# Input weights of a gated mixing network brought in by output halves, the products begun one unit sooner, and the low-rank factors loaded later

## What is computed

```python
scores = (q @ k.T) / 8 + bias            # 8 heads of 64, local window of 96 keys and 8 global keys
x = softmax(where(keep, scores, -1e9)) @ v          # then heads side by side: x is (2, 768, 512)
h = relu(x @ w_in)                                  # (512, 1024)
u, v = h[..., :512], h[..., 512:]
v_n = (v - mean(v)) / sqrt(var(v) + 1e-6)           # per token
x = (u * (w_spatial @ v_n + b_spatial)) @ w_out
u = x + V.T @ (U.T @ x)                             # along the tokens, rank 32
out = u + relu(u @ w_ch1) @ w_ch2                   # 512 -> 2048 -> 512
```

## Time and profile of the kernel before

| | |
|---|---|
| runs | 557.4, 559.49, 560.1 us |
| the profiled execution | 562.82 us, of which the span of instructions is 560.7 us |
| mean granted TensorE clock | 0.980 of full speed |
| busy, of the span | TensorE 95%, VectorE 52%, ScalarE 31%, GpSimd 20% |
| DMA | 36.25 MB, mean 65 GB/s; the q1 queue (SyncE's) 39776 packets |
| TensorE's waits listed after 118 us | 4.7 us in five groups: for VectorE's x_lo 1.6, uT_lo 1.0, gv_lo 0.9, gated 0.8, and issue 0.4 |
| first 130 us | TensorE busy 112.9 us, VectorE 95.9 us, ScalarE 75.3 us, GpSimd 41.0 us |

### The profile page before, as it was taken

How to read it: one execution, slowest core, us unless ns; L and a number is a source line. 1 busy time by engine, 2 the same in 40 slices (tenths; PEclk the granted TensorE clock), 3 DMA queues, 4 the chain that set the end, 5 groups by cost and what they waited for, 6 DMA issues and landing times.

```text
span 560.7 us, 7652 instructions
## 1 busy us (share of the span) xinstructions
PE 533.7 (95%) x2728; PEld 418.3 (75%) x2728; DVE 289.5 (52%) x845; ACT 174.3 (31%) x429; POOL 112.0 (20%) x134
## 2 busy tenths in 40 slices
PE   7688999899999999999989999999999999999996
PEld 5455666567777788878768888888888888888884
DVE  5748888857775534689822265523146524011012
ACT  4755665645555533332311101021010102101010
POOL 5884000000000001498389500000000000000000
PEclk8969999989999999999989999999999999999999
DMA  7975454545514000055223100002000002000002
GB/s 179 226 158 130 102 102 105 119 97 130 122 47 129 29 30 0 2 168 161 84 76 112 39 0 1 0 1 75 1 0 2 0 2 75 1 0 1 0 1 79
DMA packets 45835, 36.25 MB, mean 65 GB/s; under 512 B 29504, under 2 KB 39744, under 8 KB 45792
## 3 DMA queue, kind: packets, MB, share of 16 engines
q1 hardware_dynamic: 39776, 19.34, 15.6%
q0 software_dynamic: 3216, 11.63, 6.9%
q10 hardware_dynamic: 2800, 4.72, 2.9%
HBM read 32.54 MB, written 3.15 MB: 64 GB/s over the span
## 4 chain that ended last, share of the span: by engine, by line
PE 80%; DVE 10%; POOL 4%; issue 3%; DMA 2%; ACT 1%; DVEq 0%; POOLq 0%; ACTq 0%
PE ps L1255 66%; PE ps L1228 5%; PE ps L1299 4%; PE ps L1272 4%; DVE uT_first L1051 2%; DMA w_raw<-in_moe_w_in 2%; POOL win_lo L464 2%; DVE pr L923 1%; PE ps L1390 1%; POOL win_hi L462 1%; DVE uT_lo L1058 1%; DVE wspT_lo L1010 1%; DVE sc L907 1%; DVE gv_lo L991 1%; POOL small L486 0%
## 5 line engine op out<-in xcount | busy, mean ns | idle before, releaser
L1176 DVE SCALAR_TENSOR_TENSOR hT_lo<-ps,hT_hi 128x512 fp32r<-128x512 f32 x48 | 33.2, 692 | 171.4 <-ACT hT_hi L773 171.4
L773 ACT ACTIVATE hT_hi<-ps 128x512 fp32r<-128x512 f32 x48 | 28.8, 599 | 228.2 <-PE ps L1255 228.2
L597 ACT ACTIVATE pr<-sc,small 128x256 f32<-128x256 f32 (+1 forms) x96 | 46.2, 483 | 52.2 <-DVE small L907 46.8
L907 DVE CUSTOM_DVE_ANT_0 sc<-ps,bias 128x256 f32<-128x256 f32 (+1 forms) x96 | 35.0, 400 | 22.8 <-PE ps L1272 21.2
L1255 PE MATMUL ps<-win_hi,xT_hi 128*128 128x512 f32 x96 | 40.9, 427 | 0.0
L1051 DVE STREAM_TRANSPOSE ys<-tokens 32x128 f32<-32x128 f32 x128 | 38.7, 302 | 1.8
L1255 PE MATMUL ps<-uT_hi,w1a_hi 128*128 128x512 f32 x96 | 38.0, 396 | 1.0 <-DVE uT_lo L1058 1.0
L1255 PE MATMUL ps<-win_hi,xT_lo 128*128 128x512 f32 x96 | 38.5, 401 | 0.0
L1255 PE MATMUL ps<-win_lo,xT_hi 128*128 128x512 f32 x96 | 38.4, 400 | 0.0
L1255 PE MATMUL ps<-uT_lo,w1a_hi 128*128 128x512 f32 x96 | 38.1, 397 | 0.0
L1255 PE MATMUL ps<-uT_hi,w1a_lo 128*128 128x512 f32 x96 | 38.0, 396 | 0.0
(11 more groups left out here) (154 smaller groups left out, 1096.4 us busy)
## 6 DMA issues: line engine op xcount, KB each, us to landing
w_raw<-in_moe_w_ch POOLq DMA_DIRECT2D x16, 512.0 KB, 4.0
wsp<-in_moe_w_spatial ACTq DMA_DIRECT2D x12, 384.0 KB, 3.7
vn<-in_v SPq DMA_DIRECT2D x12, 256.0 KB, 3.7
out<-ys SPq DMA_DIRECT2D x12, 256.0 KB, 2.2
qk_late<-in_q SPq DMA_DIRECT2D x24, 112.0 KB, 3.5
qk_late<-in_k SPq DMA_DIRECT2D x24, 112.0 KB, 3.7
vp<-in_v SPq DMA_DIRECT2D x10, 224.0 KB, 4.5
w_raw<-in_moe_w_in POOLq DMA_DIRECT2D x4, 512.0 KB, 6.0
```

Source lines behind the costliest of these rows:

```text
L597: act.activation(pr[:, k % 3, e, 0:w], sc[:, k % 2, e, 0:w], ACT.Exp, bias=nmax[:, k % 2, e:e + 1], scale=-1.0, accum_out=sums[:, k % 3, e ...
L773: act.activation(hT[0][:, n % 2, :], h1_ps(n), ACT.Relu).then_inc(s["hT_hi"], 1)
L907: dve.tensor_tensor_reduce(out=sc[:, k % 2, e, 0:w], in0=scores_ps(k, e)[:, 0:w], in1=bias[:, 2 * p + e, WINDOW - w:WINDOW], scale=-SCALE, ...
L1176: dve.scalar_tensor_tensor(hT[1][:, n % 2, :], h1_ps(n), 0.0, hT[0][:, n % 2, :], ALU.max, ALU.subtract).then_inc(s["hT_lo"], 1)
```

## The change

w_in's four chunks are cut another way. Chunks 0 and 1 are now the upper and lower 256 rows of its second half of columns (v's), chunks 2 and 3 the same of the first half (u's). Each is loaded as two blocks of 128 rows by 512 columns, as w_out's are, and a piece is half of one such block. `LAG` is 6, so the first quarter goes into unit 6 and `ALONE` is 30. TensorE waits for the chunks one by one: for tile 0, quarter q waits for chunk q; and it waits for `xT_lo` behind the unit's transposes instead of ahead of them. U's load leaves GpSimd's queue; SyncE issues U's and V's loads at tile 4, after its keys and ahead of its values. GpSimd takes the deviations of tiles 0, 1 and 2 behind chunks 3, 4 and 5, then that of tile 3, then splits U and V, then the deviations of tiles 4 and 5. ScalarE casts V in unit 20. `qk_odd` is moved up by 3 KB, so that tile 1 of `gv_lo` is clear of it, and VectorE's wait for the turns comes one tile later. The branch for dense masks gets V's cast in another place; it does not run.

```diff
--- before.py
+++ after.py
@@ -48,7 +48,7 @@
 TURNS = P // TURN
 TILES = B * NT
 LAST = TILES * NP - 1
-LAG = 7
+LAG = 6
 ALONE = LAG + NT * NP
 SHARED = 9
 FOUR = 8
@@ -163,7 +163,7 @@
         sc_d = sb("sc_d", [P, S])
         pr_d = sb("pr_d", [P, S])
         assert place[0] <= gv_end
-        place[0] = bias_d_at
+        place[0] = bias_d_at + S * 4
         qk_odd_at = place[0]
         qk_odd = sb("qk_odd", [P, 2, NP, SPAN, TURN])
         assert place[0] <= gv_end
@@ -376,7 +376,9 @@
         def weight_chunk(name, c):
 
             if name == "in":
-                return w_in[c * P:(c + 1) * P, :], [w[:, c, :] for w in win]
+                at, n = c % 2 * 2, slice((1 - c // 2) * DM, (2 - c // 2) * DM)
+                return (w_in[at * P:(at + 2) * P, n].rearrange("(a p) n -> p a n", p=P),
+                        [w[:, at:at + 2, n] for w in win])
             if name == "ch1":
                 half, row = c // CM, c % CM
                 return (w_ch1[row * P:(row + 1) * P, half * CHUNK:(half + 1) * CHUNK],
@@ -418,7 +420,8 @@
                     (load_first if tile < 2 else load_qk)(sp, tile, a)
                 if tile == 1:
                     sp.wait_ge(s["k_loaded1"], 16)
-                if tile == 2:
+                if tile == 4:
+                    sp.dma_start(u_raw, U.rearrange("(k p) r -> p k r", p=P)).then_inc(s["u_loaded"], 16)
                     for a in range(P // RANK):
                         sp.dma_start(v4_raw[a * RANK:(a + 1) * RANK, :], V).then_inc(s["v4_loaded"], 16)
                 load_v(tile)
@@ -453,15 +456,14 @@
 
             def split_piece(n, r):
                 _, (hi, lo) = weight_chunk(*chunks[n])
-                if len(hi.shape) == 3:
-                    hi, lo = [w.rearrange("p a n -> p (a n)") for w in (hi, lo)]
-                piece = slice(r * CHUNK // PIECES, (r + 1) * CHUNK // PIECES)
-                raw = w_raw[:, n % 2, piece]
+                piece = CHUNK // PIECES
+                hi, lo = [w[:, r // 2, r % 2 * piece:(r % 2 + 1) * piece] for w in (hi, lo)]
+                raw = w_raw[:, n % 2, r * piece:(r + 1) * piece]
                 if r == 0:
                     pool.wait_ge(s[f"chunk_loaded{n % 2}"], 16 * (n // 2 + 1))
-                pool.tensor_copy(hi[:, piece], raw).then_inc(s["piece_hi"], 1)
+                pool.tensor_copy(hi, raw).then_inc(s["piece_hi"], 1)
                 pool.wait_ge(s["piece_hi"], n * PIECES + r + 1)
-                ins = pool.tensor_tensor(lo[:, piece], raw, hi[:, piece], ALU.subtract)
+                ins = pool.tensor_tensor(lo, raw, hi, ALU.subtract)
                 if r == PIECES - 1:
                     ins.then_inc(s["chunk_split"], 1)
                     pool.wait_ge(s["chunk_split"], n + 1)
@@ -510,10 +512,11 @@
             for n in range(ready["out"]):
                 for r in range(PIECES):
                     split_piece(n, r)
-                if n == 0:
-                    pool.dma_start(u_raw, U.rearrange("(k p) r -> p k r", p=P)).then_inc(s["u_loaded"], 16)
+                if n >= ready["in"] - 1:
+                    deviation(n - ready["in"] + 1)
+            deviation(3)
             split_u_v()
-            for m in range(NT):
+            for m in range(4, NT):
                 deviation(m)
             wait(pool, "qk_turned", TILES)
             for n in (ready["out"], ready["out"] + 1):
@@ -699,10 +702,11 @@
                 late_heads()
                 all_patches()
                 set_first(1, 0, q_d_turned[:, :, P:2 * P])
-                v4_hi()
                 for b in range(B):
                     wait(act, "h_ps", b * NT)
                     every_values(b)
+                    if b == 0:
+                        v4_hi()
                     load_wsp(0)
                     for p in range(NP):
                         every_pair(b, p)
@@ -737,7 +741,7 @@
                     if k in (26, 28):
                         wsp_hi(0, 0, (k - 26) // 2, False)
                     probs_out(k)
-                    if k == 6:
+                    if k == 20:
                         v4_hi()
                     if k == 8:
                         load_wsp(0)
@@ -1138,7 +1142,7 @@
                     if t >= 0 and q == 3:
                         normed(0, t)
                     if t >= 1 and q == 1:
-                        if t == 2:
+                        if t == 3:
                             wait(dve, "qk_turned", NT)
                         gv_lo(0, t - 1)
                     if k in (26, 28):
@@ -1441,7 +1445,12 @@
                         keep_busy(k, 2)
                     probs_transpose(k)
                     if between is not None:
-                        u_v_piece(0, between // NP, between % NP, False)
+                        t, q = between // NP, between % NP
+                        if t == 0:
+                            pe.wait_ge(s["chunk_split"], q + 1)
+                        if q == 0:
+                            wait(pe, "xT_lo", t + 1)
+                        u_v_piece(0, t, q, False)
                     if k:
                         probs_v(k - 1)
                     score(k + 3)
@@ -1451,11 +1460,6 @@
                 turn_first(1)
                 score(2)
                 for k in range(ALONE):
-                    t, q = (k - LAG) // NP, (k - LAG) % NP
-                    if (t, q) == (0, 0):
-                        pe.wait_ge(s["chunk_split"], ready["in"])
-                    if t >= 0 and q == 0:
-                        wait(pe, "xT_lo", t + 1)
                     unit(k, k - LAG if k >= LAG else None)
                     if k in (25, 27):
                         if k == 25:
```

## The result

The changed kernel takes 562.51 us (median of 17 runs, 559.02 to 568.22), the kernel before in the same comparison 558.98 (17 runs, 557.4 to 561.45). The ratio is 1.0054, with a 95% interval of 1.003 to 1.0079: slower by half a per cent, where 556.2 us was forecast. The ratio is taken over the runs, without one of 568.22 us that fell in the chip's slower state, and is not the quotient of the medians (1.0063).

The account below looks back on a forecast made before the run. TensorE, busy 533.7 of 560.7 us, was taken as the bound. Terms -1.8 - 1.0 - 3.3 - 2.0 + 1.5 + 1.1 + 1.3 + 0.9 gave -3.3 us, from the 559.5 median to 556.2; range 553.8 to 560.4.

Parts of the forecast that it names:

- wait for win_lo: TensorE's 1.84 us wait at 33.35 for all of w_in: would go with the new chunk order, -1.8 us.
- between my two ends: Clock term, low stretch from 29.2 us: -3.3 us, with ends 0 and -4.2.
- The keys: Tile 2's keys at the start: sooner once U's and V's loads leave it, -1.0 us (0 to 1.9).
- the rule on queues: DMA engines alternate between queues, each queue's descriptors starting in order: keys gain about nothing, total gain 1.0 us less.
- VectorE's order: Statistics in the turn's unit delay scaling and xT_lo: 0.6 us in units 10, 14, 18, 22; net +1.5 (0 to 3).
- +0.55 for each of w_out's chunks: w_out's two chunk splits, now over busy units, hold VectorE's instructions: +1.1 us together (0 to 2.5).
- V's split: V's subtraction on GpSimd, now behind tile 3's deviation, slows unit 21's norming; unit 23 late: +1.3 us (0 to 1.8).
- a gain of 2.0: TensorE's 2.02 us wait before 47.76, beside V's last split, would go: -2.0 us.
- the fourth: Rival: VectorE takes GpSimd's place; units behind the turn wait for scaling and xT_lo, 563.1 us, slower; chance 0.12.
- break-even: In the fourth rival, 0.6 us lost a tile; from 1.1 on, slower by over 0.5%.
- forecast 0.6: Tile 8's turn delays xT_lo of tile 6, which ends the 1.96 us wait: +0.6 us.

Follow-up runs that it names:

- The LAG 6 kernel with the old queue: Kernel before with w_in's halves, single-chunk waits and products begun in unit 6; U, V and deviations stay as before: 564.27 us, ratio 1.0065.
- After again: The changed kernel, unedited, run and profiled a second time: 562.35 us, ratio 1.0047 against the kernel before.
- the kernel with late statistics: Changed kernel, LAG still 6, with VectorE's statistics, norm and low part of v and ScalarE's high part one unit later: 554.52 us, ratio 0.9924.
- LAG 7: Changed kernel with the products begun in unit 7 again, all else as changed: 554.89 us, ratio 0.9927 against the kernel before.
- before again: The kernel before, unedited, profiled a second time in one run: 561.44 us.
- the halves alone: Kernel before with only w_in's halves and TensorE's single-chunk waits, LAG 7: 559.31 us, ratio 0.9982; repeated once, 559.11 us.

## Why the prediction was wrong

**What held.** No wait for win_lo is left. The clock's low stretch of 10.2 us at 29 is gone or 3.4 us long, between my two ends. Unit 11 comes 6.7 us sooner in the first pair of profiles, 4.9 in the second (3.9 from unit 0), for the 6 forecast. The keys gained less than 1.0 us: units 5 to 6 start to start, which hold that wait, average 4.4 us in the six profiles with early loads (4.1 to 5.4) and 3.8 in the eight with late ones (3.5 to 4.1), a gain of some 0.6. By the rule on queues that the prediction takes from the Trainium skill (DMA: Bandwidth & Descriptors, Queues, rings and completion order) it would be about nothing; the rows lie between that and 1.0, and the ranges touch.

**What failed: "VectorE's order", +1.5.** I counted what follows the turn by VectorE's own work, at its own durations, and got 0.6 us in each of units 10, 14, 18 and 22. GpSimd's work I priced in steps of its own, +0.55 for each of w_out's chunks and +1.3 for V's split, as if they fell anywhere. But the statistics release the deviation, and behind the deviation stand, in GpSimd's queue, exactly those chunks and V. With the statistics between turn and scaling, GpSimd starts just as VectorE does the one thing TensorE waits for, and the kernel that moves only VectorE's steps for v and ScalarE's high part of v wins all of it back: 7.8 us by the medians, some 7 by the ratios, where my terms for these three things (+1.5, +1.1, +1.3) came to 3.9. From unit starts of after, each less 3.2 us for a unit at full speed:

| units | after | over 3.2 | GpSimd beside it | forecast |
|---|---|---|---|---|
| 9 to 10 | 36.79 to 41.14 | 1.15 | chunk 4 | 0.6 + 0.55 |
| 13 to 14 | 51.00 to 55.39 | 1.19 | chunk 5 | 0.6 + 0.55 |
| 17 to 18 | 65.25 to 68.93 | 0.48 | deviation alone | 0.6 |
| 21 to 22 | 78.75 to 84.69 | 2.74 | U and V | 0.6 + 1.3 |

The units with chunks lose what was forecast, V's 0.8 more. Of the 5.6 us in these four units, VectorE's own order is some 1.9, by the 0.48 where GpSimd does a deviation alone, and the rest stands beside GpSimd's splits. The LAG 6 kernel with the old queue has 0.52, 0.47 and 0.65 us in units 13 to 14, 17 to 18 and 21 to 22, with GpSimd at 0.55 us of deviation in each. But I had set 0.3 a tile against this for what before loses, and had put losses nowhere else.

After again and the kernel with late statistics start unit 9 at 39.28 and 39.30. To unit 30 the first takes 84.2 us and the second 75.6, 8.6 us more: 1.1 in 9 to 10, 1.1 in 10 to 14, nothing in 14 to 18, 3.1 in 18 to 22, 0.8 in 22 to 26 (1.7 us of low clock among it), 0.2 in 26 to 29, and 2.2 in 29 to 30, where after again has its fall at 117.7, an estimated 1.7 us as half of 3.4. From there to TensorE's last matmul nothing is added; the two runs are 7.8 us apart (562.27 and 554.49) because the late kernel takes 0.9 us longer behind that matmul.

That V's wait of 2.4 us brings the fall behind it is argued from four profiles and not shown: both of after have wait and fall, V in four pieces (1.20 us) and LAG 7 have neither the long wait nor the fall. In the first profile of after that fall was longer, 6.8 us, of which TensorE worked 5.91: 3.0 us. I had counted the clock only as a gain, at the start, and asked nowhere what a new wait of 2 us would do to it later.

**V's split, +1.3 (0 to 1.8).** My replay put it on the norm of unit 21, which has room; it fell on the scaling. The trace of before already had this case: 2.34 us for two scalings, and 2.02 us of waiting. I took that wait away as a gain of 2.0 and put in a smaller one, where the same thing had only been moved. The row shows the scaling ending at 84.63, GpSimd's subtraction at 84.48. The Trainium skill (SBUF — State Buffer, Who interferes with whom) states that the engine which holds the pair of ports the two share keeps it for its whole instruction; the trace agrees, and the run with four pieces does too: the hold fell to 0.8 us with pieces of 0.67.

**The rivals.** The time was that of the fourth, 563.1, to which I gave 0.12. Its mechanism was the right one: the unit behind the turn waits for scaling and xT_lo. I argued against it that VectorE idles 1.48 us once a tile and catches up; it does, but what TensorE has waited by then is lost, and in 17 to 18, where GpSimd is idle, the price is 0.48, below break-even. It is GpSimd's place that carries it over. Its sum had no fall of the clock in it and five equal tiles, and came out right partly by such errors cancelling.

**The end.** xT_lo's wait is 2.47 us for 1.96, +0.5 for the forecast 0.6; the wait for ScalarE's transposed probabilities at 104.27, 1.65 us, was not foreseen; LAG 7 has 0.9 there.

**The pair of profiles.** The profiled execution of before had the long fall at 29 us, one at 114.5 and one at 288.5. The last is absent from before again. I priced the clock's gain from one execution; its median may hold less of it. How much isn't settled: the second pair of profiles is 0.8 us apart, the medians 2.3.

**Where the miss lies.** My terms ahead of unit 11 add up to -7.0 us (-1.8 - 1.0 - 3.3 - 2.0 + 0.6 + 0.55), those behind it to +3.65. Measured were -6.7 and +3.1 in the first pair of profiles (the fall at 288.5 in before flatters the second figure by an estimated 1.7), -4.9 and +5.6 in the second. The first pair thus comes out near the forecast, -3.65 us of span for -3.3, and that is luck: the execution of after lay 3.5 us below its median, that of before 3.8 above. In the second pair the start gives 2 us less than forecast and the rest costs 2 us more. What then remains of the miss isn't seen in any profile.

**What each part is worth**, by the runs: the halves alone nothing (0.9982), the deviations between the splits 2.0 us, the late loads up to 2.4 (the intervals show the 4.4 us of both together, and neither by itself), the unit sooner -5.0 with the old queue and -7.5 with the new. The change without the unit sooner is a gain of 0.7%. With the unit sooner and VectorE's statistics left behind the turn it is the same, 0.9924: the earlier pieces bring nothing of their own, within what can be measured.

## What to carry to other kernels

When a step moves on one engine, follow what its end releases on the others, and ask what those then overlap: an engine's slack is a place in its order and not a share of its time. Put work of GpSimd where it starts behind VectorE's instructions that TensorE waits for, and look for VectorE's usual instruction at an unusual duration before and after. Before pricing a removed wait, ask which queue it was hiding, and look at more than one profile of the kernel before where the clock falls.

## What the hardware showed unexpectedly

The same kernel loses its clock in different places. Between unit 0 and the last 6 us, after had 1.2 GHz at 83.6 to 90.4 us in one profile, and at 29.0 to 32.4, 87.0 to 90.4 and from 117.7 in the other, with waits of TensorE that agree to 0.4 us in each group. Over fourteen profiles a fall between 278 and 293 us, where the work is the same in all, came in seven, 3.4 or 6.8 us long, at an estimated cost of half of that.

A low clock can be free: 6.8 us of it ahead of unit 9 moved unit 12 by 0.11 us where GpSimd's queue set its time.
